# Levels 1 to 3 of a chunked scan: one 128-row product per chunk over a zero-spread r, in place of two 64-row products

## The reference, cut to what matters

```python
# attention part: B, H, S, D = 4, 8, 768, 48
for t in range(S):
    cur = einsum('bhd,bhe->bhde', u[None] * kt, vt)
    y[:, :, t] = einsum('bhd,bhde->bhe', rt, state + cur)
    state = wt[:, :, :, None] * state + einsum('bhd,bhe->bhde', kt, vt)
# then x = y as [3072, 384]; a soft mixture of 8 experts (phi, w1, w2), and
return (relu(x @ w_in) ** 2) @ w_out          # 384 -> 2048 -> 384
```

## Time and profile before

| | |
|---|---|
| median of 3 runs | 581.05 us (575.93 to 581.23) |
| the profiled execution, its own time | 576.1 us |
| its span | 574.3 us |
| mean granted TensorE clock | 0.927 |
| busy: PE, DVE, ACT | 87%, 59%, 49% |
| rounds of the attention part | from 22 to 264.5 us of the span |

### The profile page before, as it was taken

One profiled execution on the slowest core, in us unless ns is written; L12 is line 12 of the kernel. 1 busy time (PEld: TensorE's weight loads), 2 busy tenths in 40 slices (PEclk: granted clock), 3 DMA queues, 4 the chain that ended last, 5 costly groups with the idle time before them and its releaser, 6 DMA issues.

```text
span 574.3 us, 20916 instructions
## 1 busy us (share of the span) xinstructions
PE 497.8 (87%) x9002; PEld 438.8 (76%) x9002; DVE 336.1 (59%) x583; ACT 283.0 (49%) x593; POOL 12.2 (2%) x19
## 2 busy tenths in 40 slices
PE   1978898788889889767879869999999999999996
PEld 1667777677777777666733429999999999999996
DVE  5587748667676878854443236655555555555552
ACT  1544434444545455415311345666656666666653
POOL 8000000000000000000000000000000000000000
PEclk9997859779896989968989998999999999999999
DMA  6785463736536262194099932010101010100001
GB/s 112 144 203 96 141 119 88 156 62 179 102 62 110 40 108 51 24 336 130 19 322 398 369 114 99 0 43 2 42 0 43 1 41 0 42 6 35 31 12 41
DMA packets 119796, 56.37 MB, mean 98 GB/s; under 512 B 102944, under 2 KB 116256, under 8 KB 119328
## 3 DMA queue, kind: packets, MB, share of 16 engines
q1 hardware_dynamic: 116512, 42.54, 29.7%
q10 hardware_dynamic: 3200, 12.58, 6.1%
HBM read 50.38 MB, written 4.72 MB: 96 GB/s over the span
## 4 chain that ended last, share of the span: by engine, by line
PE 82%; issue 7%; ACT 5%; DVE 2%; POOL 2%; POOLq 0%; ACTq 0%; DVEq 0%
PE lbank L456 14%; PE bank L695 12%; PE bank L696 12%; PE bank L697 12%; PE tbank L399 8%; PE ybank L473 5%; PE bank L685 4%; PE ybank L489 4%; PE tbank L412 3%; PE bank L634 2%; PE bank L611 2%; PE ybank L429 2%; ACT aa L786 1%; ACT rt L731 1%; POOL rk L376 1%
## 5 line engine op out<-in xcount | busy, mean ns | idle before, releaser
L695 PE MATMUL bank<-wo_high,h_high 128*128 128x384 f32 x384 | 129.9, 338 | 2.1 <-DVE h_low L1160 1.9
L696 PE MATMUL bank<-wo_low,h_high 128*128 128x384 f32 x384 | 129.4, 337 | 0.0
L697 PE MATMUL bank<-wo_high,h_low 128*128 128x384 f32 x384 | 129.4, 337 | 0.0
L1158 DVE CAST h_high<-h_sq 128x384 fp32r<-128x384 f32 x128 | 46.0, 359 | 97.7 <-PE bank L697 89.0
L907 ACT ACTIVATE h_relu<-bank 128x384 f32<-128x384 f32 x128 | 63.0, 492 | 75.4 <-PE bank L685 75.2
L456 PE MATMUL lbank<-rk 64*64 64x32 f32 (+1 forms) x3840 | 78.5, 226 | 21.6 <-issue 20.5
L456 PEld LDWEIGHTS lbank<-rk 64*64 64x64 f32 (+1 forms) x3840 | 68.0, 140 | 37.5 <-issue 36.0
L1016 DVE COPY_PREDICATED aa<-masks,lbank 128x384 f32<-128x384 int32 (+1 forms) x80 | 59.8, 748 | 49.0 <-PE lbank L456 48.4
L995 DVE TENSOR_TENSOR rk<-rk,wl 112x768 f32<-112x768 f32 x80 | 76.4, 957 | 17.6 <-PE lbank L456 17.6
L695 PEld LDWEIGHTS bank<-wo_high,h_high 128*128 128x128 f32 x384 | 72.9, 190 | 3.3 <-issue 2.9
L1160 DVE TENSOR_TENSOR h_low<-h_sq,h_high 128x384 fp32r<-128x384 f32 x128 | 71.5, 559 | 4.5
(11 more groups left out here) (119 smaller groups left out, 472.4 us busy)
## 6 DMA issues: line engine op xcount, KB each, us to landing
w_sb<-in_moe_w_dram ACTq DMA_DIRECT2D x8, 1536.0 KB, 7.8
w_hi<-in_moe_w_dram SPq DMA_DIRECT2D x16, 384.0 KB, 8.7
nat<-in_w_dram SPq DMA_DIRECT2D x64, 72.0 KB, 2.5
nat<-in_r_dram SPq DMA_DIRECT2D x64, 72.0 KB, 2.4
nat<-in_k_dram SPq DMA_DIRECT2D x64, 72.0 KB, 2.4
v_tok<-in_v_dram SPq DMA_DIRECT2D x32, 144.0 KB, 3.4
w_lo<-in_moe_w_dram SPq DMA_DIRECT2D x1, 4608.0 KB, 16.4
out_dram<-o_sb SPq DMA_DIRECT2D x8, 576.0 KB, 3.0
```

The source lines that it names most:

```text
L695: nc.tensor.matmul(acc, hi, wo_high[:, fb, :], start=(fb == 0), stop=False)
L696: nc.tensor.matmul(acc, hi, wo_low[:, fb, :], start=False, stop=False)
L697: last = nc.tensor.matmul(acc, lo, wo_high[:, fb, :], start=False, stop=(fb == NF - 1))
```

## The change

At levels 1, 2 and 3 (`WIDE`) both heads of a slot go through one product of 128 rows. For this ACT copies the right halves of r into a new tensor `wide`, which is zero elsewhere: head 0 into its first 384 columns on partitions 0 to 47, head 1 into its second 384 columns on partitions 64 to 111 (`widen`, two copies for a level of one slot). The moving operand has 2 by 32 columns then, and a level of one slot has 12 products in place of 24. They write the first 384 columns of `lbank`, in one PSUM bank. DVE does `update` ahead of `merge` now. ACT's order is written anew: `widen` stands between the copies of the inputs, `top_level_out` of slot 0 comes ahead of `y_to_x` of slot 1, and that of slot 1 stands behind the first `widen` of the next round. Since `wide` takes room, three experts' weights are loaded early in place of four, behind `spread_w` in their round, then three late in the last round and two at its end.

```diff
-    W1_EARLY = 4
+    W1_EARLY = 3
+    WIDE = (1, 2, 3)
...
+        wide = [sb(f"wide{s}", [P, 2, S // 2], c=att) for s in range(2)]
...
-            for n, tile in enumerate(rt + rk0 + rk1 + rk2):
+            for n, tile in enumerate(rt + rk0 + rk1 + rk2 + wide):
...
+                if lv in WIDE:
+                    pe.wait_ge(widened[s], 2 * (len(WIDE) * rd + WIDE.index(lv) + 1))
+                    for c in range(NC):
+                        i, par = divmod(c, 2)
+                        dst = lbank[s][C * par:C * par + C, 0:2 * PER * SUB].rearrange("p (h x) -> p h x", h=2)
+                        last = nc.tensor.matmul(dst[:, :, SUB * i:SUB * i + SUB], src[:, 1, C * c:C * c + C],
+                                                wide[s][:, :, SUB * c:SUB * c + SUB], start=True, stop=True)
+                    last.then_inc(level_mm[s], 1)
+                    return
...
+            def widen(rd, s, lv):
+
+                m = 1 << lv
+                act.wait_ge(updated[s], 6 * rd + lv)
+                if lv > WIDE[0]:
+                    act.wait_ge(level_mm[s], 6 * rd + lv)
+                elif rd > 0:
+                    act.wait_ge(level_mm[s], 6 * (rd - 1) + WIDE[-1] + 1)
+                for h, (a, b) in enumerate(HEADS):
+                    right = rk[rd % 3][s][a:b, 0, :].rearrange("p (n two m) -> p n two m", two=2, m=m)[:, :, 1, :]
+                    nc.scalar.activation(wide[s][a:b, h, :].rearrange("p (n m) -> p n m", m=m), right, ACT.Copy)\
+                        .then_inc(widened[s], 1)
...
+                widen(rd, 0, 2)
                 if late:
                     kv_out(rd - 1, 1)
                 if ahead:
-                    inputs_out(rd + 1, 1, 6)
+                    inputs_out(rd + 1, 1, 1)
+                widen(rd, 1, 2)
+                if ahead:
+                    inputs_out(rd + 1, 2, 2)
+                widen(rd, 0, 3)
+                if ahead:
+                    inputs_out(rd + 1, 4, 2)
+                widen(rd, 1, 3)
...
+                top_level_out(rd, 0)
                 if late:
                     y_to_x(rd - 1, 1)
                 if ahead:
                     inputs_out(rd + 1, 11, 1)
-                top_level_out(rd, 0)
+                if ahead:
+                    widen(rd + 1, 0, 1)
                 top_level_out(rd, 1)
+                if ahead:
+                    widen(rd + 1, 1, 1)
                 if rd == ROUNDS - 1:
-                    load_w1(act, W1_EARLY + 3, NE)
+                    load_w1(act, NE - 2, NE)
...
+                        update(rd, s, lv)
                         merge(rd, s, lv)
-                        update(rd, s, lv)
```

More of the change, by code:

```diff
@@ L186, in fused_kernel @@
         top_out = sem2("top_out")
+        widened = sem2("widened")
         w_pair = sem("w_pair")
@@ L372, in _ @@
             pool.wait_ge(pool_const, POOL_CONSTS)
-            for n, tile in enumerate(rt + rk0 + rk1 + rk2):
+            for n, tile in enumerate(rt + rk0 + rk1 + rk2 + wide):
                 if n:
                     pool.wait_ge(rows_zero, n)
-                pool.memset(tile[96:P], 0.0).then_inc(rows_zero, 1)
+                pool.memset(tile[96:P] if n < 8 else tile[:], 0.0).then_inc(rows_zero, 1)
         @block.tensor
@@ L803, in _ @@
             inputs_out(0, 0, 12)
+            act.wait_ge(rows_zero, 10)
+            for s in range(2):
+                widen(0, s, 1)
             for rd in range(ROUNDS):
@@ L808, in _ @@
                     k_out(rd - 1, 0)
+                if late:
                     k_out(rd - 1, 1)
+                if late:
                     kv_out(rd - 1, 0)
@@ L815, in _ @@
                 if ahead:
-                    inputs_out(rd + 1, 1, 6)
[L817 to L822, removed]
+                    inputs_out(rd + 1, 1, 1)
[7 more added lines that the diff above has]
+                if ahead:
+                    inputs_out(rd + 1, 6, 1)
                 if late:
@@ L828, in _ @@
                     spread_w(rd, s)
+                if rd < W1_EARLY:
+                    load_w1(act, rd, rd + 1)
+                if rd == ROUNDS - 1:
+                    for s in range(2):
+                        act.wait_ge(updated[s], 6 * rd + 2)
+                    load_w1(act, W1_EARLY, NE - 2)
                 if ahead:
-                    inputs_out(rd + 1, 8, 3)
+                    inputs_out(rd + 1, 8, 2)
+                if ahead:
+                    inputs_out(rd + 1, 10, 1)
+                top_level_out(rd, 0)
                 if late:
@@ L1005, in merge @@
                 width = SUB if lv else C
-                data = lbank[s][:, 512 - PER * width:512 + PER * width].rearrange("p (n t) -> p n t", t=width)
+                at = 0 if lv in WIDE else 512 - PER * width
+                data = lbank[s][:, at:at + NB * width].rearrange("p (n t) -> p n t", t=width)
                 dst = aa[rd % 2][s][:]
```

## The result

| | before | after |
|---|---|---|
| median, range, executions | 581.14 us (575.93 to 582.22), 4 | 554.12 us (553.13 to 555.19), 4 |
| ratio, 95% interval | | 0.9604 (0.9556 to 0.9651) |
| profiled execution, its span | 576.1, 574.3 us | 555.19, 553.4 us |
| granted clock, busy PE, DVE, ACT | 0.927, 87%, 59%, 49% | 0.953, 88%, 60%, 60% |

The change wins 27 us between the medians, 23 us by the ratio and 20.9 us between the profiled executions. Each ratio compares executions in the same state, so the median beside it can point a little to one side.

What follows compares the result with a forecast made beforehand. TensorE was taken as the bound of the rounds, with 27.5 us of stalls without a semaphore. Terms summed to -5.9 us, giving 570.2 (profiled) or 575.2 (median); the forecast was 572 us, range 558 to 587.

Steps and rivals of the forecast that it cites:

- code: Rounds 1 to 7: 24 fewer products per wide level shrink TensorE's stalls without a semaphore, -10 us (0 to -16).
- product, change of shape: Wide levels: slightly more array time, +1.7 us; 0.12 us for each switch to 64-row products behind them, +3.4 us.
- copies, as waits on `wide`: ACT's copies into wide hidden at level 2, late by 0.5 us a round at level 3 of slot 0: +3.5 us.
- end of the round: Level 0 of slot 0 starts at once; slot 1's waits 1 us, k's second turn 0.5: -3.5 us (0 to -9).
- clock: With fewer stalls, fewer stretches fall to the lower level of 1.2 GHz: -2 us (+3 to -6).
- weights, behind the rounds: Experts' weight loads moved later are in time, but the last v and code blocks come in their company: +1 us.
- busy DMA engines make them: Code blocks in the rounds were taken to come late because of other DMAs, causing TensorE's stalls without a semaphore.
- just hidden: Level 2 of slot 1: the pair of copies ends near 217.0 us, when TensorE wants it, margin 0.
- The rival of late copies: Copies into wide end 0.8 us later at levels 2 and 3, TensorE waits 2.5 us a round: 586 to 588, chance 0.2.
- My mark for being wrong: Prediction wrong if TensorE waits over 10 us for ACT's copies, or if the stalls do not shrink.
- the mark of 0.72 to 0.80: Expected time in us of a wide level of 24 products in the changed kernel's profile.
- The marks for round 6: Expected busy times in round 6 of the changed kernel: ACT near 20 us, DVE unchanged at 22.4.

Runs made afterwards that it cites:

- half-column kernel: Changed kernel with only head 0's 32 columns in the wide product, head 1 left out at levels 1 to 3: 563.09 us; repeated on another chip, 571.88 us.
- Without the loads: Loads of r, k and w dropped from round 2 on: kernel before 572.19 us (0.9941), changed kernel 554.08 us (0.9649).
- the kernel with the most stalls: Changed kernel's orders with 64-row products and no copies into wide, all 64 columns of r at levels 1 to 3: 567.68 us (0.9789).
- orders alone: Changed kernel with the 64-row products of before at all levels and no copies into wide: 563.8 us (0.9734); again on another chip, 572.41 us (0.9843).
- the moved copy alone: Kernel before with slot 0's copy of level 5 ahead of y_to_x of slot 1: 573.51 us, too scattered for a ratio.
- the experiment that takes it back: Changed kernel with level 5 of slot 0 copied behind y_to_x and the last copies of the inputs, as before: 561.69 us (0.9733).

## Why the prediction was wrong in size

The direction was right and the size far too small. The sum was -5.9 us on the profiled execution; it came to 555.2 - 576.1 = -20.9 there, three and a half times as much. Term by term, in the profiled executions:

| term | predicted | measured |
|---|---|---|
| code | -10 | -11.6 (stalls 27.5 to 15.9) |
| product, change of shape | +1.7, +3.4 | -2 to 0 together (whole rounds at the upper level) |
| copies, as waits on `wide` | +3.5 | +8.0 |
| end of the round | -3.5 | -4.8 (`aa` -7.0, `k_tok` +2.2) |
| clock | -2 | -10 to -12 (what is left of busy -12.1) |
| weights, behind the rounds | +1 | +1.2 |
| ahead of the rounds | 0 | -2.7 |

The clock's row and that of the product come to -12.1 together. The right column sums to -22.0; the 1.1 us to -20.9 lie in small waits of the rounds that are not listed, and in rounding.

**The step that failed is the clock term**, in its size and in its cause. I took -2 us with ends of +3 and -6, although showed 35.1 us at 0.74 beside 28.4 us at 0.94 for the same 906 to 918 products. That is 29.56 against 25.39 us busy in one round, 4.2 us for 15 us less at the lower level. The windows of all seven rounds hold 69 us at the lower level; were all like round 6 (0.12 of 28.4, 3.4 us), it would be 24. At the rate of those two rounds 45 us less give 13 us. At the rate of the half-column kernel, where a round's work kept TensorE busy for 39.65 us at the lower level and 23.85 at the upper (1.66 times), they give 18. So the end of the range should have been at -13 to -18, in place of -6. It came to 40 us less and -10 to -12. The profiled execution ended 15.0 us below the sum; the clock makes 8 to 10 of them, product and change of shape 5 to 7, the first window 2.7, the stalls and the end of the round 2.9, and the waits on `wide` take 4.5 back.

**What moves the clock** I had put down to the stalls: "the clock falls with the stalls". The runs do not bear that out. Without the loads the kernel before lost a quarter of its stalls and its clock stayed at 0.910 to 0.943, and the kernel with the most stalls (36.3 us) had 0.950 to 0.962. What moved it is the columns of the products at levels 1 to 3. Two pairs of kernels, each on one chip, have the same instructions on TensorE in the same order, and differ in these columns:

| levels 1 to 3 | clock of the executions |
|---|---|
| orders alone, 32 columns, one chip | 0.916 to 0.948 |
| orders alone, 64 columns, the same chip | 0.950 to 0.962 |
| wide, 2 by 32 columns, another chip | 0.954 to 0.966 |
| wide, 32 columns, that same chip | 0.893 to 0.936 |

The 128 rows do not keep it up by themselves: the last kernel has them too. And a higher clock is not yet time: with 64 columns and the stalls in place, in the kernel before and in the orders alone, no gain in time could be told. The half columns cost 8.6 us between the two profiled executions, as much as the clock makes of the miss, but there the values differ too. That the change needed columns and fewer stalls together is my reading. Open is how much each is worth in time, what the number of instructions does at equal work, which I did not vary alone, and why the half-column kernel also has one execution at 0.969 and 553.17 us.

**Stalls of levels 1 to 3.** Right in place and nearly in size: none is left between the first product of level 1 and the turns behind level 3. That they go by the count of instructions held better than I wrote. In the traces of all the kernels here, before, changed and experiments, every distance from one stall of the rounds to the next is a multiple of 125 to 126 products, to within two: 22 distances from 125 to 504 in the kernel before, nine from 127 to 751 in the changed one. So a stall comes only where a block of some 250 instructions ends. The queue moved 60 packets for 69, and a kernel that takes a wait away gets stalls back (orders alone 33.7, the moved copy alone 33.9). That busy DMA engines make them mostly fell: without the loads 20.6 of 27.5 us remain. The Trainium skill (Runtime: NRT & Kernel Launch, Instruction fetch mechanics) calls the cost of crossing a block mostly hidden. For 27 of the 50 blocks that some 6300 products make, the trace of the kernel before agrees; at 23 TensorE stood still, and the 27.5 us, like the 15.9 that are left in the changed kernel, were not hidden.

**End of the round.** Right in kind, and 5 to 8 us by the experiment that takes it back. The forecast had the second level 0 wait 1 us each round for `aa`; it waited 0.56, 0.16 and 1.22 us in three rounds. In the other four it came late anyway, behind a stall of 1.0 to 1.7 us (three rounds) or behind a level 0 and a turn at the lower clock (one). The same move in the kernel before got most of it back as stalls. That the two parts help each other, the wide products by leaving less code to wait for, is my reading of this.

**Copies.** The place at level 3 of slot 0 was right (0.34 us), but "just hidden" at level 2 of slot 1 was wrong (0.53 us), since a pair takes 1.07 us and not 0.9. Round 7 has 0.35, 0.95 and 1.37 us. The rival of late copies had this mechanism and 2.5 us a round; it came to 1.1. My mark for being wrong, over 10 us of waits on ACT's copies, was met if all of them are counted (8.0 on `wide`, 2.2 on `k_tok`, 1.9 on `aa`), though the time went the other way. That `update` leads `merge` makes no difference that could be told. (The 588 us of this rival should read 589: 575.2 + 14.)

**Product and shape.** The wide level takes 0.85 us whatever follows, just above the mark of 0.72 to 0.80. The sum had 5.1 us for the two; by whole rounds at the upper level (23.84 us busy against 24.08 to 24.22) nothing is paid, so the second miss of the sum lies here. Where the 0.13 us a level are won back I have not found. The marks for round 6 were near enough, ACT with 21.29 us (near 20) and DVE with 22.20 (22.4).

**The first window** starts 2.7 us earlier, which no term had, since I counted from round 1 on. The trace shows 1.5 us of it in round 0 (22.30 to 44.90 before, 21.12 to 42.20 after). Before, it had stalls of 3.5 us and 1.4 us of waits on `aa`; after it has neither, but waits 1.7 and 1.0 us on `merge` and 1.6 on `wide`. The other 1.2 us lie ahead of its first product, and I have not tested why.

## What to carry to other kernels

Where TensorE's granted clock differs between like rounds, price the clock first, from the slowest and the fastest of them: here it was about half of the gain. Judge a repacked small product by the columns that it leaves in each instruction as well as by its array time, since here more columns went with a higher clock. Stalls with no releaser are worth counting out: where they stand a fixed number of instructions apart, fewer instructions in the dense stretches are the remedy that helped here. A copy that gates the next round's first product goes ahead of every copy that does not, and such a win can come back as stalls if the code there is dense.

## What was not expected of the hardware

The lower clock held for 41.0 us with TensorE busy for 39.65 of them, and for 34.0 us without any idle time, in the kernel with 32 columns in its wide products. The timeline shows the wide level at 1.43 us from its start to the next thing in the first stretch, and at 0.82 in a round at the upper level:

```profile
61.73 1.50 PE L451 MATMUL lbank<-wide,rk 128*64 128x32 f32 x24
63.16 2.80 PE L485 MATMUL ybank<-v_tok,aa 64*64 64x48 f32 x48
...
148.39 0.89 PE L451 MATMUL lbank<-wide,rk 128*64 128x32 f32 x24
149.21 0.87 PE L402 MATMUL tbank<-ident,nat 128*112 128x128 f32 x6
```

The Trainium skill (TensorE: Matmul & The Clock Gate, Part 1) has the clock set by how busy the engine has been recently. The stretches above say that what the profile counts as busy is not enough for a reader to tell the clock from: its row must be read by itself.

A product with 64 moving columns takes hardly longer than one with 32: the wide level takes 0.85 us with 2 by 32 columns and 0.82 with 32. The kernel before with all 64 columns at levels 1 to 3 takes as long as without (0.999).
